# Second down product as seven block products in place of eight, on one core

## The reference, cut to what matters

```python
x = attention(q, softmax-packed k, v, p)          # 4608 tokens x 512
h = x @ w_in                                      # 512 -> 2048
x = (max(h, 0) + alpha * min(h, 0)) @ w_out       # 2048 -> 512
g = x @ w_gate                                    # 512 -> 1536
u = g * (1 / (1 + exp(-g))) * (x @ w_val)         # 4608 x 1536
return u @ w_down                                 # 1536 -> 512
```

## Time and profile before

| | us |
|---|---|
| median of 3 runs | 1629.11 |
| profiled execution, own time | 1628.95 |
| its span, first to last instruction | 1627.1 |
| TensorE busy, share of the span | 1598.1, 98% |
| VectorE | 1015.0, 62% |
| ScalarE | 693.6, 43% |
| sets with 512 columns, one every | 12.24 |
| sets with 384 columns, one every | 9.36 |

### The profile page before, as it was taken

The page is one execution under the profiler, slowest core; times in us unless marked ns, Lnnn a source line. Parts: engine busy times, 40 slices in busy tenths (PEclk is TensorE's granted clock), DMA queues, the critical chain, the costliest instruction groups (busy, mean ns, idle before and its releaser), DMA issues.

```text
span 1627.1 us, 24548 instructions
## 1 busy us (share of the span) xinstructions
PE 1598.1 (98%) x9510; PEld 1468.5 (90%) x9510; DVE 1015.0 (62%) x1888; ACT 693.6 (43%) x1481; POOL 47.4 (3%) x81
## 2 busy tenths in 40 slices
PE   8999999999999999999999999999999999999999
PEld 5899988999999999999988888888888889999999
DVE  5776679867798768877544464444644454446443
ACT  4565567555675557645422132222312232223122
POOL 0000000100000000010000000000000000000000
PEclk9999999999999999999999999999999999999999
DMA  7343224433333324343454433544164435563561
GB/s 263 117 125 110 71 82 160 162 115 96 123 93 126 123 79 135 130 151 138 125 202 158 159 117 115 190 149 165 62 206 143 140 113 200 186 207 103 203 202 39
DMA packets 99219, 227.05 MB, mean 140 GB/s; under 512 B 9744, under 2 KB 37408, under 8 KB 99104
## 3 DMA queue, kind: packets, MB, share of 16 engines
q1 hardware_dynamic: 90624, 194.02, 36.7%
q0 software_dynamic: 8480, 31.47, 5.0%
HBM read 184.56 MB, written 40.89 MB: 139 GB/s over the span
## 4 chain that ended last, share of the span: by engine, by line
PE 80%; DVE 13%; ACT 3%; issue 2%; DMA 1%; SPq 0%; ACTq 0%; DVEq 0%
PE acc L880 9%; PE acc L672 8%; PE acc L674 8%; PE acc L673 8%; PE h L672 7%; PE side L672 7%; PE h L674 7%; PE h L673 7%; PE side L674 7%; PE side L673 7%; PE acc L884 5%; DVE piece L1304 3%; DVE mixed L1304 2%; DVE floats L1489 2%; DVE g L1304 1%
## 5 line engine op out<-in xcount | busy, mean ns | idle before, releaser
L880 PE MATMUL acc<-g,w 128*128 128x288 f32 x1792 | 272.4, 294 | 0.0
L880 PEld LDWEIGHTS acc<-g,w 128*128 128x128 f32 x1792 | 248.9, 188 | 0.0
L995 ACT ACTIVATE g<-floats 128x288 fp32r<-128x288 f32 x256 | 113.8, 444 | 224.2 <-DVE floats L1489 139.0
L1304 DVE TENSOR_TENSOR g<-floats,g 128x288 fp32r<-128x288 f32 x256 | 115.0, 449 | 76.5 <-ACT g L995 75.3
L672 PE MATMUL h<-attn,mixed 128*128 128x288 f32 x512 | 157.5, 308 | 3.5 <-DVE floats L1489 2.2
L1489 DVE SCALAR_TENSOR_TENSOR floats<-floats,h 128x288 f32<-128x288 f32 x256 | 130.2, 509 | 43.8 <-ACT floats L1157 42.0
L884 PE MATMUL acc<-g,w 128*128 128x288 f32 x896 | 156.1, 296 | 0.2 <-DVE g L1304 0.2
L674 PE MATMUL h<-attn,mixed 128*128 128x288 f32 x512 | 151.0, 295 | 0.0
L673 PE MATMUL h<-attn,mixed 128*128 128x288 f32 x512 | 150.9, 295 | 0.0
L1304 DVE TENSOR_TENSOR piece<-floats,piece 128x512 fp32r<-128x512 f32 (+3 forms) x203 | 135.6, 688 | 23.1 <-ACT piece L995 20.7
L1304 DVE TENSOR_TENSOR u<-sums,u 128x512 fp32r<-128x512 f32 (+1 forms) x120 | 76.6, 638 | 91.1 <-ACT u L995 91.1
(11 more groups left out here) (277 smaller groups left out, 3682.6 us busy)
## 6 DMA issues: line engine op xcount, KB each, us to landing
ring<-w_scratch SPq DMA_DIRECT2D x90, 512.0 KB, 5.7
ring_c<-w_scratch SPq DMA_DIRECT2D x60, 512.0 KB, 5.1
w_scratch<-piece POOLq DMA_DIRECT2D x36, 512.0 KB, 4.0
floats<-w_in SPq DMA_DIRECT2D x64, 256.0 KB, 3.2
ring_b<-w_scratch SPq DMA_DIRECT2D x30, 512.0 KB, 7.0
y_scratch<-floats POOLq DMA_DIRECT2D x16, 576.0 KB, 3.5
floats<-kT SPq DMA_DIRECT2D x28, 288.0 KB, 2.9
floats<-qT SPq DMA_DIRECT2D x28, 288.0 KB, 2.9
```

The costliest lines, as they stand in the source:

```text
L880: pe.matmul(acc[:, m, 0:CH], w2[:, j, x, m * P:(m + 1) * P], g[:, s % 2, 0, :], start=False, stop=False)
L995: return nc.scalar.activation(dst, src, ACT.Copy, **kw)
L1304: return nc.vector.tensor_tensor(dst, x, high.bitcast(F32), ALU.subtract)
```

## The change

The down product is done by the same seven-product scheme as gate and value. The contraction (1536 rows, in 6 pairs of tiles) and the output (512 columns, in two halves of 256) are cut in two, and so are the tokens (the two halves of a run). For each of the 6 pairs, u gives four blocks B11, B12, B21, B22, from which T1 to T4 are summed. This makes 7 x 6 = 42 tiles a run, each with 2 output blocks: 6 matmuls a tile. `TILES` gives their order: B11 and T1 of each pair run beside sets 1 to 11 (`down_tile(r, j - 1)`), all others after the sets.

- u is kept unsplit in SBUF (`u_of`), where w_down was. Sums T1 to T4 of u are made in place by DVE (`sum_of_u`). A ring of 6 tiles holds the split halves (`tile_hi` on ACT, `tile_lo` on DVE): single tiles beside the sets, pairs (2 x 512 columns in one instruction) after them. Block steps after the sets also take both k blocks in one instruction.
- The split block sums of w_down are made in layer one as six more kept sets (18 in place of 12), and POOL writes them to d_scratch in 7 DMAs a set, 256 KB each. The twelve "d" splits are gone. KEEP_AT is spread anew, and a set takes four slots in a row (offsets 0, 1, 2, 3 in place of 0, 1, 3, 4).
- SP streams d_scratch to SBUF, one 256 KB DMA a tile, into a ring of 5 (`load_tile`): tile t when tile t-5 has been used. It now stands in SP's queue between the weights of the sets, with stores and y loads spread one to a set.
- Output: the 7 partial products meet in banks and four fp32 buffers (`copy_lead`, `copy_fifth`, `out_two`, `out_three`, `out_12`, `out_22`, `out_21`, `out_11`); one 2-block store per quarter.

```diff
-KEEP_AT = [62, 73, 79, 97, 117, 141, 162, 181, 202, 208, 214, 220]
+KEEP_AT = [62, 72, 76, 80, 97, 117, 121, 137, 141, 162, 181, 200, 204, 208, 212, 216, 220, 224]
-    for _i, _off in enumerate((0, 1, 3, 4)):
+    for _i, _off in enumerate((0, 1, 2, 3)):
-for _j in range(NT2):
-    MID[LAST + NT1 + 3 + _j].append(("split", ("d", _j)))
+AFTER_SETS = [("tile", 16), ("T4", 0), ("tile", 18), ("block", T_ORDER[0]), ("tile", 20), ("T4", 2), ("tile", 22),
...
+            def load_tile(t):
+                if t >= WRING:
+                    once.wait_ge(tile_done, t - WRING + 1)
...
+                sp.dma_start(tile_weights(t).bitcast(F32), dS[k, part, side_by]).then_inc(tile_landed[t % WRING], 16)
...
+            for r in range(RUNS):
+                for j in range(NT2):
+                    n = NT2 * r + j
+                    if 1 <= j <= 4 and r:
+                        store(r - 1, (11, 22, 21, 12)[j - 1])
+                    if n + 1 < SETS and (j or r == 0):
+                        load_weights(n + 1)
...
+                    if j:
+                        load_tile(NTILES * r + j - 1 + WRING)
+                    if 5 <= j < 5 + KD and r + 1 < RUNS:
+                        load_y(r + 1, [j - 5])
+                for i in range(BESIDE - 1, NTILES):
+                    load_tile(NTILES * r + i + WRING)
+                    if r + 1 < RUNS and i in (14, 18, 22, 26):
+                        load_weights(NT2 * (r + 1) + 1, [(i - 14) // 4])
...
+                    if e[1] >= NT2:
+                        for s in range(1 if e[2] == 0 else 2):
+                            pool.dma_start(dS[e[1] - NT2, e[2], s], piece(p)[:, :, 256 * s:256 * s + 256].bitcast(F32)
+                                           ).then_inc(kept[e[2]], 16)
...
-                for m in range(KD):
...
-                    mm = product(bank_groups[(r + 1 + half) % 2][m][:, 0:h],
-                                 hl(lambda x: down(j)[:, x, m * P:(m + 1) * P]),
-                                 hl(lambda x: u_high_low[:, d % 2, x, 0:h]), j == 0, j == NT2 - 1,
+                w, x = tile_weights(t), made_of(i)[:, i % 2, :, :]
+                for m in range(2):
+                    mm = product(part_banks[name][m][:, 0:h], hl(lambda a: w[:, a, m * P:(m + 1) * P]),
+                                 hl(lambda a: x[:, a, 0:h]), k == 0 and name not in ("B21", "B22"), k == PAIRS - 1,
```

More of the change, by code:

```diff
@@ L385, in build @@
         yraw = f(4096, 2 * KD * HW).rearrange("p (k c n) -> p k c n", k=KD, c=2)
[L386 to L392, removed]
+        first_term, first_two = [rows_a[:, i * HW:(i + 1) * HW] for i in range(2)]
+        first_three, silu1 = [rows_b[:, i * HW:(i + 1) * HW] for i in range(2)]
+        lead, fifth, two, three = [f(2 * i * HW, 2 * HW).rearrange("p (m n) -> p m n", m=2) for i in range(4)]
         side = ctx.enter_context(nc.psum_tensor("side", [P, 2, 512], F32))
@@ L572, in load_y @@
                     once.wait_ge(attnF_ready, NCH - 1)
+                    once.wait_ge(piece_split, len(PIECES))
                 once.wait_ge(y_stored, 16 * min(NCH, -(-(START_OF[r] + 2 * HALF[r]) // CH)))
-                for k in range(KD):
+                for k in ks:
                     sp.dma_start(yraw[:, k, :, 0:HALF[r]],
@@ L664, in _ @@
             for i in range(4):
-                once.wait_ge(kept[i], 16 * NT2)
+                once.wait_ge(kept[i], kept_by(i, NKEEP - 1))
         @block.tensor
@@ L1001, in left @@
                 if e[0] == "keep":
-                    once.wait_ge(kept[e[2]], 16 * (e[1] + 1))
+                    once.wait_ge(kept[e[2]], kept_by(e[2], e[1]))
                 elif e[0] == "scores1" and last:
@@ L1234, in _, with out_11 @@
+            def out_11(r):
+                once.wait_ge(tile_done, NTILES * r + TILE_NO["B21", PAIRS - 1] + 1)
+                once.wait_ge(two_of_out, r + 1)
+                copy(lead[:, :, 0:HALF[r]], acc[:, 0:2, 0:HALF[r]]).then_inc(out_ready[11], 1)
             for e in PLAN:
@@ L1283, in _ @@
                         copy_first(n)
+                    if j:
+                        tile_hi(r, j - 1)
+                    if j == NT2 - 2:
+                        tile_hi(r, BESIDE)
+                    elif j == NT2 - 1:
+                        tile_hi(r, BESIDE - 1)
+                        tile_hi(r, BESIDE + 2)
                     silu_1(n)
-                    u_hi(2 * NT2 * r + j)
                     if j == NT2 - 1:
-                        u_hi(2 * NT2 * r + NT2)
+                        copy_lead(r)
                     silu_2(n)
-                for j in range(NT2):
-                    if j + 1 < NT2:
-                        u_hi(2 * NT2 * r + NT2 + j + 1)
-                    if j == 1:
-                        out_copy(2 * r)
-                    if r + 1 < RUNS:
-                        for step in T_STEPS[2 * j:2 * j + 2]:
-                            block_step_high(r + 1, step)
-                out_copy(2 * r + 1)
+                copy_fifth(r)
+                for e in AFTER_SETS:
+                    if e[0] == "tile":
+                        tile_hi(r, e[1])
+                    elif e[0] == "block" and r + 1 < RUNS:
+                        block_step_high(r + 1, e[1])
+                    elif e == ("out", 11):
+                        out_11(r)
         @block.vector
@@ new lines, in out_two, with out_three @@
+            def out_two(r):
+                h = HALF[r]
+                once.wait_ge(tile_done, NTILES * r + TILE_NO["T2", PAIRS - 1] + 1)
+                once.wait_ge(lead_copied, r + 1)
+                once.wait_ge(out_stored[12], 16 * r)
+                nc.vector.tensor_tensor(two[:, :, 0:h], side[:, :, 0:h], lead[:, :, 0:h], ALU.add
+                                        ).then_inc(two_of_out, 1)
+            def out_three(r):
+                h = HALF[r]
+                once.wait_ge(tile_done, NTILES * r + TILE_NO["T3", PAIRS - 1] + 1)
+                once.wait_ge(two_of_out, r + 1)
+                once.wait_ge(out_stored[21], 16 * r)
+                for m in range(2):
+                    nc.vector.tensor_tensor(three[:, m, 0:h], hb[m][:, 0:h], two[:, m, 0:h], ALU.add
+                                            ).then_inc(three_of_out, 1)
@@ L1630, in _ @@
                 elif e[0] == "tstep":
[L1631 removed]
+                    block_step_low(0, e[1], slice(e[2], e[2] + 1))
                 elif e[0] == "set0":
```

452 lines of the change are left out of this document (280 added, 172 removed).

## The result

The changed kernel takes 1624.12 us (median of 11 runs, 1621.15 to 1629.83), the kernel before in the same session 1629.29 (11 runs, 1628.23 to 1630.7): ratio 0.997, 95% interval 0.9958 to 0.9981. It gains 5 us where 11 were forecast. The runs of the changed kernel scatter over 8.7 us, those of before over 2.5. The profiled execution took 1622.99 us, its span 1621.1.

A forecast was written before the change was run, and what follows sets the result against it. TensorE, busy 98% at full clock, was taken as the bound: matmuls times their pace, plus waits. 1628.95 - 37.0 (matmuls) + 16 (weights) + 2 (tiles) + 7 (layer one) + 1 (end) = 1618 us, range 1598 to 1640.

The forecast's parts named there:

- Matmuls, -37.0: Layer two: 36 fewer matmuls in each run, 24.5 us saved in 512 runs and 12.5 in 384 runs, all on the path.
- Layer one, +7: Six added kept sets: three covered, three at 2 us each, plus 1 us for a piece behind a chunk store.
- Three fall into stretches where VectorE is already at: Layer one: three added sets in stretches where VectorE would reach 96 to 98% busy, priced 2 us each, 6 us.
- The piece behind a chunk store: Layer one, slot 210: a piece's write behind a chunk store makes ScalarE wait 1.5 us, 1 us of it reaching TensorE.
- if layer two starts after 835: Sign: layer two was to start near 823 us instead of 815; after 835 the layer one step is wrong.
- Weights late in 384 sets, +16: Layer two, 384 runs: weight bursts land in 8.25 us, later behind tiles and stores, against 8.13 allowed; 16 us, ends 4 and 30.
- Tile loads, +2: After the sets: 512 KB weight loads between tile loads in run 4 delay tiles; 2 us, between 0 and 6.
- VectorE in layer two, 0: Splits and sums keep up beside the matmuls, tightest in the last set; taken as 0, at most 3 us.
- the end, +1: Kernel's end: the last sum covers 768 columns in place of 384, then one 384 KB store; 1 us more.
- Rival 1: Layer two: weight bursts land within 8.13 us, so 16 + 2 us go; 1596 us, up to 1606; chance 0.25.
- Rival 2: Each added kept set stalls TensorE in layer one; at 6.4 us a set it ends at 1649 us; chance 0.14.
- Rival 3: After the 384-column sets, streamed tiles land in 4.3 us rather than 3.1, 20 us more, 1636 us; chance 0.12.

The follow-up runs named there:

- experiment 10: Kernel of experiment 7, but the four weight DMAs of the next run's second set are issued in that run's first set, not among tile loads: 1599.03 us, ratio 0.9812.
- experiment 3: Changed kernel, but POOL issues a layer-one chunk's store after the kept writes of the next four slots: 1622.39 us, ratio 0.9955.
- Experiment 4: Changed kernel with kept sets at the old slots up to 181, then ten in a row from slot 200; block steps 12 slots later: 1611.43 us, ratio 0.9895.
- experiment 1: Changed kernel with layer one's old twelve kept sets; down-weight sets left out, other pieces written instead, output not the reference's: 1608.02 us, ratio 0.9864.
- experiment 6: Changed kernel with the next run's four weight DMAs among the tile loads put seven tiles apart in place of four: 1625.03 us, ratio 0.9969.
- experiment 8: Changed kernel with one kept set moved from slots 72 to 83 to the end, the two left there in old slots: 1619.68 us, ratio 0.9938.
- experiment 7: Changed kernel with the edits of Experiment 4, experiment 5 and experiment 6 together: 1603.33 us, ratio 0.9833.
- experiment 5: Changed kernel with one semaphore for each of a set's four weight DMAs, so a term waits only for its part: 1614.65 us, ratio 0.9907.
- experiment 2: Changed kernel with runs of 464, 464, 464, 464 and 448 columns in place of 512 and 384: 1623.63 us, ratio 0.9965.

## Why the prediction was wrong

The profiled execution lies 5 us over the forecast: layer one was 10.7 too small, the weights' term 7.3 too large, the tiles' 1.4 too small, and 0.2 is assigned to nothing. That the total is only 5 us off is luck: two errors of 10.7 and 7.3 us went opposite ways.

- **Matmuls, -37.0:** right. The 512 runs shrank by 8.1 us each (3 x 36 x 0.2267 in all), with no wait, as the 122-us window shows; experiment 10 shows the rest in the 384 runs.
- **Layer one, +7: the step that failed.** Measured +17.7, the clock's 2.7 us (next point) among them. "Three fall into stretches where VectorE is already at" 86 to 88%, "I take 2 us for each": slots 60 to 92 alone, with one added set and the closer spacing, cost 7.1 us, slots 136 to 148 with another 3.1. "Three of the added sets ... fall where VectorE has room and are covered": slots 117 to 124 cost 4.0, slots 200 to 224, with one of the three priced at 2 us as well, 3.4. The piece behind a chunk store was priced at 1 us at slot 210; experiment 3 finds nothing there, and 5.5 us in slots 60 to 92. The mechanism was named, and its own test ("if layer two starts after 835") puts 833 just short of failing; the size was off by 2.5. What misled is the busy share: it did not tell where a set is covered. Experiment 4 shows it: same work, other slots, 12.7 us less; and three sets in slots 228 to 239 are free. That a set's dependent steps (piece, split, place in the ring) met no free time of VectorE in their own slots, though it had 12 to 14% free on average, is the likely reason; only for slots 60 to 92 is the chain read from the trace. The full 4.15 us of VectorE a set, from the earlier trace rows, would have given 25 us: an upper price, nearer to 17.7 than 7 was.
- **What the prediction did not have: the clock.** With a wait of 3.4 us the granted clock fell to 1.2 GHz for 6.8 us, and 2.7 us more were lost. The Trainium skill (TensorE: Matmul & The Clock Gate, Part 1: The HAM clock gate) says that the gate follows how busy TensorE has lately been; the trace agrees, since the fall at 321.2 us lies inside that wait. Falls of 3.4 us show at other places in the profiles of experiments 1, 3, 4, 6 and 8, each with a wait of 1.9 to 2.3 us, and in that of 7 after one of 1.2 us. Not every such wait has one (2.4 us at 452 us in experiment 6, without a fall), and experiment 10, whose longest wait after slot 60 is 1.5 us, shows none. The runs' mean granted clocks point to a part of the scatter: the five runs of the changed kernel at 0.999 took 1621.2 to 1624.1 us, the six at 0.997 or 0.998 took 1623.0 to 1629.8.
- **Weights late in 384 sets, +16:** the mechanism was right (first term released by the weights' DMA, sets of 8.3 to 9.7 us, cured by experiment 5), the size was 8.7. What the step left out is that a wait helps the set after it: each set was priced by itself, but the next request does not wait for the late set, so the next burst has the wait's time more. The four 384 sets from 1348.80 on last 9.44, 8.43, 9.44 and 8.43 us, though the bursts asked for in them land after 9.21, 9.23, 9.20 and 8.63; of 20 sets 7 waited, where the sum had all priced. The bursts that were waited for landed 8.8 to 9.4 us after their first request, once 10.2, against the 8.1 that the forecast allowed them.
- **Tile loads, +2:** about 3.4, for the most part from the weight loads between them, as the step said; experiment 10.
- **VectorE in layer two, 0; the end, +1:** right. No down tile waits for VectorE; the only waits for it are four of 0.3 us, each in the first set of a run. The last sum is one instruction of 0.96 us:

```profile
1617.25 0.96 DVE L1734 TENSOR_TENSOR floats<-acc,floats 128x768 f32<-128x768 f32 x1 [2.61 <-PE acc L756]
```

**The rivals.** Rival 1 (loads keep up) is wrong, by the waits for ring_b; but a small edit, four semaphores, gives its gain without faster loads. Rival 2 had the right place: at 17.7 us for six sets the mean price is 3 us a set, between the forecast's 1.2 and its 6.4. Rival 3 fell: streamed tiles land in 3.0 us.

## What to carry to other kernels

Work added to a helper engine with 12% free time in a stretch is not covered by an average: take its full busy time as the upper price until the timeline shows a gap at the very slots, and try it where TensorE waits least. A load that is just late can be split by who reads which part: here that gave 9.5 us and spreading the loads gave nothing. Where requests do not wait for the reader, as here, lateness is not paid at each of them. And a wait of TensorE can bring the slower clock with it: here one of 3.4 us cost 6.1.

## What was not expected of the hardware

- With a wait of 3.44 us the granted clock was halved for 6.8 us, 2.7 us of extra time; at the same place in experiments 2 and 5 a wait of 3.8 us halved it for 3.4 us.
- The pace of matmuls is not one line in the columns: 173.3 ns at 384 and 226.7 at 512, but 194.9 at 432, 202.0 or 207.6 at 448, 209.0 at 464 and 217.0 at 480, where the line between them gives 193.3, 200.0, 206.7 and 213.3.
- A 256 KB load issued 0.67 us behind a single 512 KB load took 6.0 us, twice the median of 3.0, with a DMA share of 0.93 between 1448 and 1455 us (experiment 7).
